# One core, eight batches of attention and gated MLP: a part's tile steps in a new order

## What is computed

```
kv  = k^T v per head;  o = q kv;  x = o / rms(o) * g_norm          # 8 heads of 64
logits = x w_gate; the best 2 of 4 experts, softmax of their logits = w
per expert e: a = causal softmax(x wq_e (x wk_e)^T / 8);  y = sum over e of w_e (a x wv_e) wo_e
h = gelu(y w_in);  u, v = halves of h (512 each);  v = layernorm(v) * g_ln
vs = w_sg v + b_sg (over the tokens);  out = y + (u * vs) w_out
```

## Time and profile before

| | before |
|---|---|
| median of 3 executions | 866.47 us (863.19 to 866.83) |
| the profiled execution | 863.27 us, its span 861.4 us |
| mean granted TensorE clock | 0.994 of full |
| TensorE matmuls busy | 818.8 us (95%), 6637 instructions |
| weight loads busy | 730.1 us (85%) |
| DVE / ACT / POOL busy | 493.4 (57%) / 361.9 (42%) / 188.3 us (22%) |
| DMA, mean over the span | 55 GB/s |

### The profile page before, as it was taken

How to read it: one execution, slowest core, us unless ns; L and a number is a source line. 1 busy time by engine, 2 the same in 40 slices (tenths; PEclk the granted TensorE clock), 3 DMA queues, 4 the chain that set the end, 5 groups by cost and what they waited for, 6 DMA issues and landing times.

```text
span 861.4 us, 16863 instructions
## 1 busy us (share of the span) xinstructions
PE 818.8 (95%) x6637; PEld 730.1 (85%) x6637; DVE 493.4 (57%) x1289; ACT 361.9 (42%) x827; POOL 188.3 (22%) x243
## 2 busy tenths in 40 slices
...
DMA packets 117406, 47.29 MB, mean 55 GB/s; under 512 B 94352, under 2 KB 110736, under 8 KB 117328
## 3 DMA queue, kind: packets, MB, share of 16 engines
...
...
## 4 chain that ended last, share of the span: by engine, by line
PE 72%; DVE 15%; ACT 7%; issue 3%; POOL 2%; DMA 0%; DVEq 0%; ACTq 0%; POOLq 0%
PE w L1012 33%; PE t L1012 18%; PE t L1073 4%; PE t L1155 3%; ACT probs L685 3%; PE t L1058 3%; PE w L1043 3%; DVE w L800 3%; PE t L1140 2%; PE t L1163 2%; PE w L1110 2%; PE w L1209 2%; DVE squares L853 2%; ACT L707 1%; DVE work L942 1%
## 5 line engine op out<-in xcount | busy, mean ns | idle before, releaser
L1012 PE MATMUL w<-wout_s,big 128*128 128x512 f32 x432 | 108.1, 399 | 1.3 <-DVE big L843 0.5
L1012 PE MATMUL w<-wsgT_s,big 128*128 128x288 f32 x768 | 107.0, 295 | 0.0
L1012 PE MATMUL t<-big,wqk_s 128*128 128x288 f32 x768 | 105.3, 296 | 0.2 <-issue 0.2
L1012 PEld LDWEIGHTS w<-wsgT_s,big 128*128 128x128 f32 x768 | 103.6, 188 | 0.0
L1012 PEld LDWEIGHTS t<-big,wqk_s 128*128 128x128 f32 x768 | 102.5, 188 | 0.4 <-issue 0.4
L1012 PEld LDWEIGHTS w<-wout_s,big 128*128 128x128 f32 x432 | 79.6, 188 | 20.0 <-DVE big L843 2.9
L800 DVE CUSTOM_DVE_ANT_0 w<-w,causal 128x64 f32<-128x64 f32 (+4 forms) x160 | 75.4, 516 | 33.5 <-PE w L1043 32.0
L582 POOL TENSOR_TENSOR yT<-squares,yT 128x256 fp32r<-128x256 f32 (+1 forms) x32 | 22.3, 698 | 314.6 <-ACT yT L699 314.6
L1012 PE MATMUL t<-w_s,yT 128*128 128x512 f32 x240 | 65.5, 414 | 6.3 <-POOL yT L582 4.5
L713 ACT ACTIVATE big<-work 128x576 fp32r<-128x576 f32 x32 | 22.0, 686 | 110.7 <-POOL work L609 95.3
L967 DVE SCALAR_TENSOR_TENSOR work<-w,gln_c,bias_t 128x576 f32<-128x576 f32 x32 | 26.2, 818 | 70.7 <-PE w L1012 70.0
...
## 6 DMA issues: line engine op xcount, KB each, us to landing
...
```

Of the source, the lines that this page charges most:

```text
L1012: last = nc.tensor.matmul(o, stationary(hs, c), mv(hm, c), start=c == of[0] and p == 0, stop=c == of[-1] and p == len(PASSES) - 1)
```

## The change

The list of a part gets a new order, and the bank table follows it. From T0 on TensorE's list is now, in parts 1 to 6: T0 T1 s4 s5 pv0 pv1 KV s6 s7 T2 pv2 pv3 v4 s8 T3 pv4 pv5 s9 h0 h1 pv6 pv7 T4 h2 pv8 pv9 h3 u0 (first half) h4 u0 (second half). Parts 0 and 7 keep v4 before pv0; part 0 keeps KV at the end, part 7 has none. The first gate group (ranks, exponentials, weights) moves ahead of the second half of the queries and keys; the second group's ranks move from before `scale 3` to after T3's copies, and its exponentials ahead of exponential 9. Exponential 7 now comes after the first copy of T2, which goes from DVE to ACT (the second goes the other way). In part 0 the turned blocks of w_sg are spread anew. Tiles 0 to 3 and tile 4 of yT now count on semaphores of their own (`yT_lo`, `yT_last`). The diff (the line that names the new semaphore is left out):

```diff
@@ -84,16 +84,18 @@
 
 
     T_UNITS = {t: [4] * (t + 1) if t < NT - 1 else [8, 8, 4] for t in range(NT)}
-    T_SLOT = {0: ["t0"], 1: ["t1", "t2"], 2: ["t3", "t1", "t2"], 3: ["t3", "t1", "t2", "t0"], 4: ["w0", "w1", "t3"]}
-
-    T_DVE = {(1, 0), (2, 0), (2, 2), (3, 1), (3, 3), (4, 0), (4, 2)}
-    Y_SLOT = {0: "t0", 1: "t0", 2: "t3", 3: "t0", 4: "t0"}
+    T_SLOT = {0: ["t0"], 1: ["t1", "t2"], 2: ["t1", "t2", "t3"], 3: ["t2", "t3", "t0", "t1"], 4: ["w0", "w1", "t2"]}
+
+    T_DVE = {(1, 0), (2, 1), (2, 2), (3, 1), (3, 3), (4, 0), (4, 2)}
+    Y_SLOT = {0: "t0", 1: "t0", 2: "t2", 3: "t1", 4: "t0"}
 
     GATES = [(0, 4), (4, NT)]
 
     def tile_scores(t):
 
         return [("s", 2 * t), ("s", 2 * t + 1), ("exp", 2 * t), ("exp", 2 * t + 1)]
+
+    KV = [("kv", c) for c in range(DC)]
 
     def copies(t, *among):
         return [("T_copy", (t, i)) for i in among]
@@ -101,7 +103,7 @@
     def values(t):
         return [("pv", 2 * t), ("pv", 2 * t + 1), ("y_mul", t), ("yhi", t)]
 
-    def attention(first):
+    def attention(first, last):
 
         def late(*units):
             return list(units) if first else []
@@ -109,30 +111,27 @@
         plan = [("qk", (0, 0))] + late(("split", "wqk1")) + [("qk", (EP, 0))] + late(("split", "wqk3"))
         plan += [("qk", (1, 0))] + late(("split", "wv")) + [("qk", (EP + 1, 0))] + late(("w2e", 0))
         plan += [("v", 0)] + late(("w2e", 1), ("v", 1), ("double", 0)) + tile_scores(0)
-        plan += ([("wsgT", 0), ("v", 2)] if first else [("v", 1), ("v", 2)]) + tile_scores(1) + late(("wsgT", 1)) + [("v", 3)]
-        plan += [("qk", (0, 1)), ("ranks", 0), ("qk", (EP, 1)), ("g_exp", 0), ("weights", 0), ("scale", 0), ("qk", (1, 1)),
-                 ("scale", 1)] + late(("split", "wo")) + [("qk", (EP + 1, 1)), ("T", 0), ("T", 1)]
-        plan += copies(0, 0) + copies(1, 0, 1) + tile_scores(2) + [("v", 4), ("scale", 2)] + values(0)
-        plan += tile_scores(3) + [("T", 2)] + copies(2, 0, 1, 2) + [("ranks", 1), ("scale", 3)] + values(1)
-        plan += [("s", N - 2), ("T", 3)] + copies(3, 0) + [("exp", N - 2)] + copies(3, 1, 2, 3)
+        plan += ([("v", 2)] if first else [("v", 1), ("v", 2)]) + tile_scores(1) + [("v", 3)]
+        plan += [("ranks", 0), ("g_exp", 0), ("weights", 0), ("qk", (0, 1)), ("scale", 0), ("qk", (EP, 1)), ("scale", 1),
+                 ("qk", (1, 1))] + late(("split", "wo")) + [("qk", (EP + 1, 1)), ("T", 0), ("T", 1)]
+        plan += copies(0, 0) + copies(1, 0, 1) + tile_scores(2) + ([("v", 4)] if first or last else [])
+        plan += [("scale", 2)] + values(0) + ([] if first or last else KV)
+        plan += [("s", 6), ("s", 7), ("T", 2), ("exp", 6)] + copies(2, 0) + [("exp", 7)] + copies(2, 1, 2) + [("scale", 3)] + values(1)
+        plan += late(("wsgT", 0)) + ([] if first or last else [("v", 4)])
+        plan += [("s", N - 2), ("T", 3)] + copies(3, 0) + [("exp", N - 2)] + copies(3, 1, 2, 3) + [("ranks", 1), ("g_exp", 1)]
         return plan + values(2) + [("s", N - 1), ("exp", N - 1)]
 
-    ATTENTION = attention(False)
-
-
-    def mlp(first, last):
-        plan = [("h", 0), ("g_exp", 1), ("weights", 1), ("scale", NT - 1), ("h", 1), ("gelu", 0), ("gelu", 1)] + values(3)
-        plan += [("T", 4)] + copies(4, 0, 1, 2) + [("h", 2), ("h", 3), ("pv", N - 2), ("pv", N - 1), ("gelu", 2),
-                 ("y_mul", NT - 1), ("yhi", NT - 1)]
-        if first:
-            plan += [("wsgT", 2), ("wsgT", 3), ("gelu", 3), ("wsgT", 4), ("wsgR", 0)]
-        elif last:
-            plan += [("gelu", 3)]
-        else:
-            plan += [("gelu", 3)] + KV
-        return plan + [("h", 4), ("gelu", 4)]
-
-    KV = [("kv", c) for c in range(DC)]
+
+    def mlp(first):
+
+        def late(*units):
+            return list(units) if first else []
+
+        plan = [("h", 0), ("weights", 1), ("scale", NT - 1), ("h", 1), ("gelu", 0), ("gelu", 1)] + values(3)
+        plan += [("T", 4)] + copies(4, 0, 1, 2) + late(("wsgT", 1)) + [("h", 2), ("pv", N - 2), ("pv", N - 1), ("gelu", 2), ("h", 3),
+                 ("y_mul", NT - 1), ("yhi", NT - 1), ("gelu", 3)] + late(("wsgT", 2))
+        return plan + [("u_half", 0), ("h", 4), ("gelu", 4)]
+
     MIX = [("u", m) for m in range(FC)] + [("vs", 0), ("vs", 1), ("turn", 0), ("vs", 2), ("turn", 1), ("turn", 2), ("vs", 3), ("turn", 3)]
 
     MIXED = [("out_y", 0), ("out_y", 1), ("o", 0), ("out_g", 0), ("o", 1), ("out_g", 1), ("o", 2), ("x", 0),
@@ -148,19 +147,22 @@
         return 1 - part % 2
 
     VHAT_AFTER = {("gelu", 2): 0, ("gelu", 3): 1, ("gelu", 4): 2, ("u", 0): 3, ("u", 1): 4}
-    QK_NTH = {j: r for r, j in enumerate(j for kind, j in ATTENTION if kind == "qk")}
-    MIX_FIRST = [x for m in range(FC) for x in (("u", m), ("wout", m))] + MIX[FC:] + KV
-    PLAN = {-1: FIRST, 0: attention(True) + mlp(True, False) + MIX_FIRST + MIXED_ONE}
-    PLAN.update({b: ATTENTION + mlp(False, False) + MIX + (MIXED if b % 2 else MIXED_ONE) for b in range(1, B - 1)})
-    PLAN[B - 1] = ATTENTION + mlp(False, True) + [x for x in MIX if x[0] != "turn"] + [x for x in MIXED if x[0] in ("out_y", "out_g")]
+    QK_NTH = {j: r for r, j in enumerate(j for kind, j in attention(False, False) if kind == "qk")}
+    LATE_U = {0: [("wsgT", 3)], 1: [("wsgT", 4), ("wout", 0)], 2: [("wsgR", 0), ("wout", 1)], 3: [("wout", 2), ("wout", 3)]}
+    MIX_FIRST = [x for m in range(FC) for x in [("u", m)] + LATE_U[m]] + MIX[FC:] + KV
+    PLAN = {-1: FIRST, 0: attention(True, False) + mlp(True) + MIX_FIRST + MIXED_ONE}
+    PLAN.update({b: attention(False, False) + mlp(False) + MIX + (MIXED if b % 2 else MIXED_ONE) for b in range(1, B - 1)})
+    PLAN[B - 1] = attention(False, True) + mlp(False) + [x for x in MIX if x[0] != "turn"] + [x for x in MIXED if x[0] in ("out_y", "out_g")]
     PREPARED = [x for part in (-1, 0) for x in PLAN[part] if x[0] in ("split", "w2e", "wsgT", "wsgR", "wout")]
 
     SLOT = {("qk", (0, 0)): "t0", ("qk", (EP, 0)): "t1", ("qk", (1, 0)): "t2", ("qk", (EP + 1, 0)): "t3",
             ("v", 0): "t0", ("v", 1): "t1", ("v", 2): "t2", ("v", 3): "t3", ("v", 4): "t3",
             ("qk", (0, 1)): "t0", ("qk", (EP, 1)): "t1", ("qk", (1, 1)): "t2", ("qk", (EP + 1, 1)): "t3",
-            ("h", 0): "t1", ("h", 1): "t2", ("h", 2): "t1", ("h", 3): "t2", ("h", 4): "t0", ("kv", 0): "t3"}
-    SLOT_FIRST = {**SLOT, ("wsgT", 0): "t3", ("wsgT", 1): "t0", ("wsgT", 2): "t3", ("wsgT", 3): "t1", ("wsgT", 4): "t2",
-                  ("wsgR", 0): "t3", ("qk", (0, 1)): "t1", ("qk", (EP, 1)): "t2", ("qk", (1, 1)): "t0"}
+            ("h", 0): "t3", ("h", 1): "t0", ("h", 2): "t3", ("h", 3): "t1", ("h", 4): "t2", ("kv", 0): "t3"}
+    SLOT[("v", 4)] = "t1"
+    SLOT_FIRST = {**SLOT, ("wsgT", 0): "t1", ("wsgT", 1): "t1", ("wsgT", 2): "t3", ("wsgT", 3): "t0", ("wsgT", 4): "t1",
+                  ("wsgR", 0): "t3", ("v", 4): "t3"}
+    SLOT_LAST = {**SLOT, ("v", 4): "t3"}
 
 
     def ring_start(part):
@@ -181,7 +183,7 @@
     def units(part):
 
         turn, got = [ring_start(part)], []
-        slots_of = SLOT_FIRST if part == 0 else SLOT
+        slots_of = SLOT_FIRST if part == 0 else SLOT_LAST if part == B - 1 else SLOT
 
         def ring(unit, among):
             if part < 0:
@@ -207,6 +209,9 @@
             elif kind == "kv":
                 if j == 0:
                     got.append((("kv", 0), slots_of[("kv", 0)] if part >= 0 else FIRST_SLOT[("kv", 0)]))
+            elif kind == "u_half" or (kind, j) == ("u", 0):
+                if kind == "u_half":
+                    got.append((("u", 0), WIDE[0]))
             elif kind in ("u", "vs", "woT"):
                 got.append(((kind, j), WIDE[j % 2]))
             elif kind == "out_y":
@@ -845,8 +851,12 @@
 
                 def y_scaled(t):
                     x = src(("y", t))[:, 0:2 * P].rearrange("p (e n) -> p e n", e=EP)
-                    if count(part, NT, t) > 1:
-                        dve.wait_ge(yT_lo, count(part, NT, t - 1))
+                    if t >= 2:
+                        dve.wait_ge(yT_lo, count(part, NT - 1, t - 1))
+                    elif t == 1 and part > 0:
+                        dve.wait_ge(yT_lo, count(part, NT - 1, 0))
+                    elif part > 0:
+                        dve.wait_ge(yT_last, part)
                     spread = pT[t % 2][:, 0:P * E * (t + 1)].rearrange("p (e a n) -> p e a n", e=EP, a=2)
                     for a in range(2):
                         rows = slice(HD * a, HD * (a + 1))
@@ -858,7 +868,7 @@
                     dve.wait_ge(yT_hi, count(part, NT, t + 1))
                     nc.vector.tensor_tensor(yT[:, LO, :, P * t:P * (t + 1)],
                                             y_t[t % 2].rearrange("p (e n) -> p e n", e=EP),
-                                            as_f32(yT[:, HI, :, P * t:P * (t + 1)]), ALU.subtract).then_inc(yT_lo, 1)
+                                            as_f32(yT[:, HI, :, P * t:P * (t + 1)]), ALU.subtract).then_inc(yT_last, 1)
 
                 to_scale = None
```

(17 more changed lines are left out.)

1 line of the change is left out of this document (added).

## The result

| | before | after |
|---|---|---|
| median of the runs | 866.65 us (863.19 to 867.22, 4 runs) | 851.91 us (849.10 to 852.01, 4 runs) |
| profiled execution | 863.27, span 861.4 | 849.1, span 847.3 |
| mean granted TensorE clock there | 0.994 | 0.998 |
| matmuls busy | 818.8 | 810.5 |

A forecast was written before the change was run, and what follows sets the result against it. TensorE was taken to bound the kernel except at four waits a part on the VectorE/ScalarE softmax chain. Waits 6 x 1.4 + 2.1 + 2.0 = 12.5 and clock 5.1: 866.5 - 12.5 - 5.1 = 848.9, so 849 us, range 840 to 860.

The forecast's parts named there:

- 1.6, taken as 1.4: Parts 1 to 6: 1.6 us worked out as saved by h4, taken as 1.4 a part, between 0.8 and 2.2.
- a wait before u3, or before the first `vs`: Sign of being wrong in kind: TensorE waits there because the chain behind gelu is late; no size given.
- its terms: Part 7: s8's wait stays, T3's 0.9 goes, pv8 waits 1.4, h4's 1.9 goes; 2.1 us saved.
- 2.0 is saved: Part 0, without KV: 2.0 us saved, after giving 1.4 back for crowded turned blocks of w_sg.
- I give 1.4 back: Part 0: 1.4 us allowed for four turned w_sg blocks between u's products, each with splits on ScalarE and VectorE.
- Nothing: KV's loads: Listed as costing nothing: KV comes 25 us earlier, its reload equally so, and its loads have a part's length of time.
- Five falls to two, 5.1: TensorE's clock: with less idle time in one place, two falls are expected in the median, not five; 5.1 us gained.
- The two rules: Skill rules: 1.38 us drain per table switch (pv8's wait 2.6, forecast 860), not followed; frequent short idles can swing the clock.
- 1: Rival, whole kernel: all waits go, covered by v4, KV, h3 and u0, with the clock's 5.1; 828 us, chance 0.06.
- 2: Rival, VectorE/ScalarE chain swallows it: T4's copies end 2.0 late, a part saves 0.3; 864 us, chance 0.10.
- 3: Rival, clock: it falls once in every part, 13.6 us for some 8.5 now; 859 us, chance 0.13.
- 4: Rival, slower: the clock falls twice in every part, after v4's and pv8's waits, 27.2 us; 873 us, chance 0.04.

The follow-up runs named there:

- e8: The changed kernel with the first gate group (ranks, exponentials, weights) back between the second-half queries and keys: 855.51 us, ratio 0.989.
- e1: The changed kernel with the first copy of T2 on ScalarE ahead of exponential 6 instead of between 6 and 7: 847.83 us, ratio 0.979.
- e4: The changed kernel with KV alone put back behind pv9, in the MLP stage, in parts 1 to 6: 860.24 us, ratio 0.994.
- e6: The changed kernel with h3 back ahead of pv8, as before the change: 858.90 us, ratio 0.992.
- e2: The changed kernel with the second gate group's ranks and exponential moved behind maximum 9 and exponential 9: 849.35 us, ratio 0.981.
- e9: The changed kernel with part 0 alone in the order and banks of the kernel before: 850.42 us, ratio 0.983.
- e11: The kernel before with only the second gate group's ranks and exponential moved behind T3's copies: 857.73 us, ratio 0.992.

## Why the forecast held, and what in it did not

**Part 1 came out as written.** Counted from T0, in us:

| | forecast | found |
|---|---|---|
| T0 to T1; s4 earlier by | 0.5; 0.45 | 0.44; 0.55 |
| maximum 6 starts | 7.7 | 7.6 |
| v4 starts; its wait | 10.4; 1.0 | 10.4; 1.01 |
| T3 starts | 13.0 | 13.0 |
| T4's copy ends | 27.1 | 27.1 |
| pv8 starts; its wait | 27.2; 1.2 | 27.3; 1.31 (parts 2 to 6: 1.12 to 1.16) |
| h4 starts | 31.8 | 31.95 |
| a middle part saves | 1.6, taken as 1.4 | 1.2 and 1.4 |

T1's wait is gone, which e8 ties to the gate group. s8's and T3's are gone, and v4's has come at the size and place named; e1 shows it to be the copy between exponentials 6 and 7, e4 that without KV another 0.94 would stand before s6. pv8's wait is there, and e6 shows what h3 covers. The table load was to come 0.7 later by the ranks (1.0 less the gate exponential and the earlier row scale). It does, 20.51 us behind T0 for 19.82 before, but the ranks are only part of the reason: with them out of the way (e2) it comes at 20.10, 0.4 sooner. Without them maximum 9 has to wait for its scores, which in part 1 end only 0.56 before it starts now (184.06 for 184.62). At h4 of part 1 1.45 of the 1.6 worked out is there, and 1.23 at the part's end.

The forecast named a wait before u3, or before the first `vs`, as a sign that it was wrong in kind. Both came. u3 waits 0.16 in seven parts for ScalarE (L715), part of what is lost behind h4, and small; the first `vs` waits 1.19, but in part 0 alone. Part 7 saved 2.7 for 2.1, not by its terms: s8's wait grew from 1.56 to 2.15, pv8's is 0.75 and not 1.4.

**Part 0 was wrong, in two steps.** "2.0 is saved" came out as 3.7 lost. The first step is the crowding of the turned blocks of w_sg, for which "I give 1.4 back": the forecast looked at their splits, but not at the places they go to. TensorE in part 0 after the change:

```profile
69.50 0.63 PE L1129 MATMUL t<-ident,vin 128*128 128x128 f32 x4 [1.00 <-ACT work L700]
74.02 0.66 PE L1068 MATMUL t<-ident,staged 128*128 128x128 f32 x4 [0.76 <-DVE wsgT_s L906]
...
86.16 0.66 PE L1129 MATMUL t<-ident,vin 128*128 128x128 f32 x4 [1.40 <-DVE squares L863]
...
99.56 0.52 PE L1134 MATMUL t<-ident,qin 64*128 64x64 f32 x5
...
103.08 0.77 PE L1232 MATMUL w<-wsgT_s,big 128*128 128x288 f32 x4 [1.19 <-DVE wsgT_s L910]
...
120.16 2.55 PE L1150 MATMUL t<-vin,kin 128*64 128x64 f32 x80 [1.92 <-DMA vin<-in_v_dram]
```

The first block (L1129) takes v4's place and its wait, its copy delays T3's last unit (0.76), the second waits 1.40 for its bank, and the first `vs` 1.19 for the last split. The second step is "Nothing: KV's loads". The last block of w_sg (L1134) is read out of `qin`, and SP's load of the q blocks waits for it. It moved from before h4 to between u2 and u3, from 94.81 to 99.56, and SP with it. SP's queue in before, and after:

```profile
95.37 8.66 SPq L442 DMA_DIRECT2D qin<-in_q_dram  x16
...
109.25 0.63 SPq L425 DMA_DIRECT2D vin<-in_v_dram  x1
```

```profile
100.12 9.45 SPq L448 DMA_DIRECT2D qin<-in_q_dram  x16
...
111.03 0.63 SPq L431 DMA_DIRECT2D vin<-in_v_dram  x1
```

v is issued 1.8 later, behind q blocks that are still being moved, and KV, which had no wait, has 1.92. From the first `vs` to KV it is 17.1 us for 15.0, so 2.1 of the 3.7 belong to this second step and the other 1.6 to the first. In e9, where the last block and the q blocks keep their old place, KV doesn't wait.

**The clock.** Five falls to two, 5.1, was the forecast for the medians, and from 0.988 or 0.990 to 0.996 over 860 us is 5.2 to 6.9. The profiled executions show three falls before and one after. One stretch of each, before and then after:

```profile
690.00:700.00 10.00, 8.78 (x72) 7.60 (x73) 8.06 (x27) 4.47 (x12) 1.47 (x2) 0.83 0.01 2
```

```profile
780.00:790.00 10.00, 10.00 (x84) 8.34 (x83) 8.39 (x32) 6.20 (x14) 1.48 (x2) 0.83 0.01 2
```

The one after lies in part 7, just behind s8's wait there (v4 keeps its old place in that part):

```profile
779.33 1.06 PE L1053 MATMUL w<-big 64*128 64x288 f32 x12 [2.15 <-ACT staged L691]
```

The reason given, "less idle time in one place", is what e11 bears out for the middle parts, and e6 too. As far as these rows go, the idle time in one place can be two waits or one: the falls of the middle parts of before stand behind s8's and T3's, this one behind a single wait.

**So the time was right in part by luck.** Of 12.5 us of waits, 7.8 + 2.7 - 3.7 = 6.8 were found, 5.7 too few. That the profiled execution took 849.1, the forecast's own number for it, is chance: two falls fewer instead of one (2.1 more than forecast), the start of part 0 (1.4) and the `vs` (1.8), neither of them forecast, and 0.3 without a place made it up. The median is 2.9 above the forecast. The start of part 0 and the `vs` are read from one execution of each kernel: the 61.14 of before looks like scatter, since e11, which has the same work up to there, is at 59.76.

**The two rules.** The table load at 187.16 takes 1.28 and the gelu starts 0.02 behind its end, as before the change. The drain of about 1.38 us that the Trainium skill, ScalarE: Activation LUTs, section What ACT_TABLE_LOAD costs, adds to each switch doesn't show, and pv8's wait is 1.31, not 2.6. As to the clock, three waits of 0.87 to 1.03 in part 1 leave it at 1.0 in the profiled execution of e6, whose other middle parts have three of 0.81 to 1.10. The Trainium skill, TensorE: Matmul & The Clock Gate, section A second HAM failure mode: psum-queue depth-cycling, warns of frequent short idles. By e6 and e11 it is rather idle time in one place that counts here, not how many waits there are; the rows behind this are at the end.

**The rivals.** 1 fell because of v4 and pv8; 2 because T4's copies end 0.7 late, not 2.0 (27.07 us behind T0 for 26.39); 3 and 4 because the clock didn't fall in the middle parts of the profiled execution, and the mean of 0.996 in the others leaves room for two falls, not eight.
